# Attention ahead of two expert layers: GpSimd's low halves in pairs, projections two groups together, result turns ahead of both outputs

## The reference

```python
def _attn_ref(q, k, v, omega):              # q, k, v: 4 x 8 x 576 x 64, omega: 128 x 64
    scale = 1.0 / np.sqrt(np.sqrt(D))
    q_s, k_s = (q * scale, k * scale)
    def phi(x):
        proj = np.einsum('bhsd,md->bhsm', x, omega)
        h = proj - np.sum(x * x, axis=-1, keepdims=True) / 2.0
        h = h - np.max(h, axis=-1, keepdims=True)
        return np.exp(h) / np.sqrt(m)
    q_p, k_p = (phi(q_s), phi(k_s))
    kv = np.einsum('bhsm,bhsd->bhmd', k_p, v)
    z = np.sum(k_p, axis=2)
    num = np.einsum('bhsm,bhmd->bhsd', q_p, kv)
    den = np.einsum('bhsm,bhm->bhs', q_p, z)[..., None] + 1e-06
    return num / den
# x = attention, 2304 x 512
# x = (h * sigmoid(1.702 h)) @ w_out, h = x @ w_in      (512 -> 2048 -> 512)
# x = top-1 of 8 experts, relu(x @ w1[e]) @ w2[e]        (512 -> 1024 -> 512)
```

## Time and profile before

| | us |
|---|---|
| median of 3 runs | 808.28 (808.04 to 808.32) |
| the profiled execution | 808.37 |
| its span | 806.3 |
| unit 0 and the start, to the first `sums` | 12.56 |
| rest of step 0 | 9.94 |
| step 1 | 8.19 |
| loop, steps 2 to 13 | 109.04 |
| steps 14 and 15 to the first matmul of the next part | 13.21 |
| the two following parts | 653.4 |

### The profile page before, as it was taken

One profiled execution on the slowest core, in us unless ns is written; L12 is line 12 of the kernel. 1 busy time (PEld: TensorE's weight loads), 2 busy tenths in 40 slices (PEclk: granted clock), 3 DMA queues, 4 the chain that ended last, 5 costly groups with the idle time before them and its releaser, 6 DMA issues.

```text
span 806.3 us, 15801 instructions
## 1 busy us (share of the span) xinstructions
PE 776.8 (96%) x5514; PEld 711.9 (88%) x5515; DVE 361.1 (45%) x908; ACT 307.6 (38%) x714; POOL 322.1 (40%) x280
## 2 busy tenths in 40 slices
PE   7999989999999999999999999999999999999995
PEld 6777777889899989988989998997999999999994
DVE  5777777511224424433443445766763322331321
ACT  3777776633232232232233223253214324425320
POOL 5777776135322222212222223234026716627521
PEclk9999999999999999999999999999999999999998
DMA  8776674011050020010002001051062541621011
GB/s 298 288 253 229 240 267 158 1 53 53 1 183 0 1 78 0 0 49 29 0 0 78 0 0 40 21 199 33 28 221 77 162 144 47 216 72 39 29 59 31
DMA packets 25444, 74.17 MB, mean 92 GB/s; under 512 B 3120, under 2 KB 3632, under 8 KB 25280
## 3 DMA queue, kind: packets, MB, share of 16 engines
q1 hardware_dynamic: 22144, 63.68, 22.6%
q0 software_dynamic: 3264, 10.03, 4.1%
HBM read 61.11 MB, written 12.58 MB: 91 GB/s over the span
## 4 chain that ended last, share of the span: by engine, by line
PE 83%; ACT 4%; POOL 4%; issue 4%; DVE 3%; DMA 1%; SPq 0%; POOLq 0%; ACTq 0%; DVEq 0%
PE pj L701 25%; PE nm L883 16%; PE pj L1301 8%; PE kv L883 8%; PE kv L1317 6%; PE nm L1317 6%; PE nm L1301 5%; POOL sqt L205 2%; POOL sqt L201 2%; ACT feat L417 1%; PE pj L255 1%; PE pj L1330 1%; PE kv L273 1%; PE tr L1288 1%; ACT qfT L397 1%
## 5 line engine op out<-in xcount | busy, mean ns | idle before, releaser
L857 POOL TENSOR_TENSOR gl<-g,gh 128x384 fp32r<-128x384 f32 x96 | 99.2, 1036 | 306.6 <-ACT gh L719 306.6
L714 DVE TENSOR_TENSOR g<-pj,sg 128x384 f32<-128x384 f32 x96 | 53.5, 557 | 220.1 <-ACT sg L709 219.8
L709 ACT ACTIVATE sg<-pj 128x384 f32<-128x384 f32 x96 | 47.2, 492 | 254.1 <-PE pj L701 254.1
L701 PE MATMUL pj<-xh,win_h 128*128 128x384 f32 x384 | 129.5, 337 | 1.2 <-DVE xl L736 1.2
L701 PE MATMUL pj<-xh,win_l 128*128 128x384 f32 x384 | 129.4, 337 | 0.0
L701 PE MATMUL pj<-xl,win_h 128*128 128x384 f32 x384 | 128.9, 336 | 0.0
L701 PEld LDWEIGHTS pj<-xh,win_h 128*128 128x128 f32 x384 | 72.1, 188 | 5.2 <-DVE xl L736 1.5
L701 PEld LDWEIGHTS pj<-xl,win_h 128*128 128x128 f32 x384 | 72.1, 188 | 3.6
L701 PEld LDWEIGHTS pj<-xh,win_l 128*128 128x128 f32 x384 | 72.0, 188 | 0.0
L1301 PE MATMUL pj<-xTh,W 128*128 128x288 f32 x320 | 71.6, 303 | 0.0
L825 DVE SCALAR_TENSOR_TENSOR raw<-tr,xT 128x512 f32<-128x512 f32 x90 | 58.6, 688 | 8.2 <-DVE g L714 7.6
(11 more groups left out here) (255 smaller groups left out, 1695.4 us busy)
## 6 DMA issues: line engine op xcount, KB each, us to landing
wraw<-in_moe_w SPq DMA_DIRECT2D x7, 2048.0 KB, 10.9
ve<-in_v_z SPq DMA_DIRECT2D x16, 585.0 KB, 3.8
qk<-in_qk_n SPq DMA_DIRECT2D x16, 576.0 KB, 5.0
qkT<-in_qk_t SPq DMA_DIRECT2D x15, 576.0 KB, 5.4
y_rows<-ys SPq DMA_DIRECT2D x18, 256.0 KB, 2.3
stage<-in_moe_w_in SPq DMA_DIRECT2D x8, 512.0 KB, 6.2
y_early<-ys SPq DMA_DIRECT2D x12, 256.0 KB, 2.7
stage<-in_moe_w_out SPq DMA_DIRECT2D x4, 512.0 KB, 6.6
```

The lines of the kernel that those rows point to most:

```text
L701: mm = eng.matmul(ph[f % 3][:, 0:BT], w[f // F1A][:, c, f % F1A, :], x[:, c, :], start=(c == 0 and w is win_h and x is xh), stop=(c == DC ...
L709: eng.activation(sg[f % 2][:, :], ph[f % 3][:, 0:BT], ACT.Sigmoid, scale=1.702).then_inc(a_sg, 1)
L714: eng.tensor_tensor(g32[f % 2][:, :], ph[f % 3][:, 0:BT], sg[f % 2][:, :], ALU.mult).then_inc(v_g, 1)
L857: eng.tensor_tensor(gl[f % 3][:, :], g32[f % 2][:, :], gh[f % 3][:, :].bitcast(F32), ALU.subtract).then_inc(g_gl, 1)
```

## The change

- SyncE: unit 0's normal layout also comes in three pieces of 192 KB, each behind the piece of the turned layout of the same group. Both layouts of unit 1 come before the values of units 0 and 1. A load of `qk` waits no longer for VectorE's sums of the unit two before (`v_sq`) but for GpSimd's first squaring of it (`g_s0`, `g_sq`).
- GpSimd: in an even step only `squares`; in an odd one `squares` and then both `low` of the two steps.
- TensorE: `project(1)` directly behind `project(0)` and ahead of `sums`; all three `turn_x` ahead of both outputs; 5, 3 and 2 idle matmuls in place of 4, 4 and 4.
- ScalarE: in even steps from 2 on `copy_x(1)` and `copy_qf(2)` go ahead of `exps_b(1)`, and `copy_x(2)` ahead of `exps_a(1)`.
- VectorE: `norms` goes from the end of step i (for unit i + 2) into `front`, behind the first `top` of the unit that uses it.

```diff
@@ sync @@
+            if isinstance(i, int) and i == 2:
+                eng.wait_ge(g_s0, PG)
+            elif not isinstance(i, int) or i > 2:
+                eng.wait_ge(g_sq, 4 * (i - 3) + 1 if isinstance(i, int) else 4 * i - 11)
-            need(eng, v_sq, i - 1)
...
+        def first(g):
             n = GT * P
             eng.dma_start(qkT[0][:, GT * g:GT * g + GT, :].rearrange("p t c -> p (t c)"),
                           qk_t[0, :, g * n:(g + 1) * n]).then_inc(ld_0[g], 16)
+            n = 2 * GT * HD
+            eng.dma_start(qk[0][:, 2 * GT * g:2 * GT * (g + 1), :].rearrange("p j d -> p (j d)"),
+                          qk_n[0, :, g * n:(g + 1) * n]).then_inc(ld_1[g], 16)
...
+        eng.dma_start(om_r[:, :], om_2).then_inc(ld_om, 16)
+        for g in range(PG):
+            first(g)
+        load(1, 0, 1, None)
         for i in (0, 1):
-            load(i, 0, i, None)
+            values(i, i)
@@ gpsimd step @@
-            if chunk is not None:
-                low(i, n, a, chunk)
+            if chunk is not None and a == 1:
+                low(2 * n, n, 0, chunk)
+                low(i, n, 1, chunk)
@@ tensor @@
-        idle(4)
+        idle(5)
...
-        idle(4)
+        idle(3)
         project(0, 0, 0, 2)
-        idle(4)
+        idle(2)
@@ tensor step @@
             project(*x, 0)
+            project(*x, 1)
             sums(i, n, a)
-            project(*x, 1)
...
-            output(i, n, a, 0)
             if before:
                 turn_x(n - 1, 2, i)
+            output(i, n, a, 0)
             output(i, n, a, 1)
@@ scalar step @@
             copy_qf(i, n, a, 1, before)
+            if before:
+                copy_x(n - 1, 1)
+                copy_qf(i, n, a, 2, before)
             exps_b(*x, 1)
             if before:
-                copy_x(n - 1, 1)
-            copy_qf(i, n, a, 2, before)
+                copy_x(n - 1, 2)
+            else:
+                copy_qf(i, n, a, 2, before)
             exps_a(*x, 1)
-            if before:
-                copy_x(n - 1, 2)
@@ vector front @@
             if w:
                 denom(*w, 0)
+            if not isinstance(x[0], int) or x[0]:
+                norms(*x)
             top_h(*x, 0)
@@ vector step @@
-                else:
-                    norms(*y)
```

More of the change, by code:

```diff
@@ L113, in attention @@
     ld_om = sem("ld_om")
-    ld_0 = [sem(f"ld_0{g}") for g in range(PG)]
+    ld_0, ld_1 = ([sem(f"ld_{b}{g}") for g in range(PG)] for b in range(2))
     g_id = sem("g_id")
@@ L142, in load @@
         def load(i, n, a, chunk):
-            if isinstance(i, int) and i == 0:
-                eng.dma_start(om_r[:, :], om_2).then_inc(ld_om, 16)
-                first_t(0)
-            need(eng, v_sq, i - 1)
+            if isinstance(i, int) and i == 2:
+                eng.wait_ge(g_s0, PG)
+            elif not isinstance(i, int) or i > 2:
+                eng.wait_ge(g_sq, 4 * (i - 3) + 1 if isinstance(i, int) else 4 * i - 11)
             eng.dma_start(qk[a][:, :, :].rearrange("p j d -> p (j d)"),
@@ L152, in load, with values @@
             need(eng, p_pj, PG * (i - 1))
-            if isinstance(i, int) and i == 0:
-                for g in range(1, PG):
-                    first_t(g)
-            else:
-                eng.dma_start(qkT[a][:, :, :].rearrange("p t c -> p (t c)"),
-                              qk_t[bass.ds(i, 1), :, :].rearrange("i p r -> (i p) r")).then_inc(ld_t[a], 16)
+            eng.dma_start(qkT[a][:, :, :].rearrange("p t c -> p (t c)"),
+                          qk_t[bass.ds(i, 1), :, :].rearrange("i p r -> (i p) r")).then_inc(ld_t[a], 16)
             if chunk is not None:
                 weights(i - 2, a, chunk)
+            if not (isinstance(i, int) and i == 1):
+                values(i, a)
+        def values(i, a):
             need(eng, p_kv, i - 1)
@@ L163, in load @@
                           v_z[bass.ds(i, 1), :, :].rearrange("i p r -> (i p) r")).then_inc(ld_v[a], 16)
-        def first_t(g):
+        def first(g):
             n = GT * P
@@ L197, in squares @@
         def squares(i, n, a):
-            eng.wait_ge(ld_qk[a], 16 * (n + 1))
+            need(eng, ld_qk[a], 16 * (n + a))
             need(eng, g_sq, 4 * i - 4)
@@ L221, in step @@
                 squares(i + 2, n + 1, a)
-            if chunk is not None:
-                low(i, n, a, chunk)
-        eng.wait_ge(ld_qk[0], 16)
+            if chunk is not None and a == 1:
+                low(2 * n, n, 0, chunk)
+                low(i, n, 1, chunk)
         for g in range(PG):
+            eng.wait_ge(ld_1[g], 16)
             t = slice(2 * GT * g, 2 * GT * (g + 1))
@@ L583, in step @@
         def step(i, n, a, last):
-            w, x, y = (i - 1, n + a - 1, 1 - a), (i + 1, n + a, 1 - a), (i + 2, n + 1, a)
+            w, x = (i - 1, n + a - 1, 1 - a), (i + 1, n + a, 1 - a)
             if not last:
@@ L604, in vector @@
         front((0, 0, 0), None)
-        norms(1, 0, 1)
         half_steps(eng, step)
```

## The result

| | before | changed |
|---|---|---|
| median, beside each other (7 and 7 runs) | 808.28 | 803.79 (803.37 to 807.05) |
| a second time (7 and 4 runs) | 807.95 | 804.07 (803.68 to 804.17) |
| ratio, with its 95% interval | | 0.9961 (0.995 to 0.9973); second time 0.995 (0.9934 to 0.9967) |

Three of its seven first runs took 805.8 to 807.1 us, at a mean granted clock of 0.991 or 0.992, and four took 803.4 to 803.8 at 0.995 or 0.996. The profiled execution of that set was the slowest of them (807.05, span 805.2); one profile more, of the second set, has a span of 802.3. I use the second for the times of the stages, and the first for its clock and for one even step (its steps agree with those of the second to 0.01 us).

What follows compares the result with a forecast made beforehand. TensorE was taken to bound the attention loop, busy 99.8 of 109.0 us. The terms - 2.2 - 1.7 + 2.1 + 0.1 + 0.3 = - 1.4 us, on a span of 806.3, gave a median of 806.9 us, range 805.4 to 809.0.

Steps and rivals of the forecast that it cites:

- even steps: about nothing: Attention loop, even steps: 1.7 us gained from the division's wait, set against 2.1 us lost by the third result turn.
- The wait for the division: Even steps: TensorE's waits for VectorE's last division go, through GpSimd's paired lows and the moved norms; gain 1.7 us.
- The third turn: Even steps: the third result turn waits 0.38 us for a copy, 1.30 from turn to turn; loss 2.1 us.
- `project(1)` in odd steps: Odd steps: it needs the even step's last exponentials earlier, with slack 0.05 us; loss 0.1 us for all.
- Rival (c): Odd steps: ScalarE ends the last exponentials late and the two projections stop TensorE; up to 810.0 us, chance 0.11.
- The end: Last steps: the split of the first block stands behind a later third copy; loss 0.3 us.
- The start: Ahead of step 1: step 1 starts at 20.3 us and not 22.50; gain 2.2 us, bounds 0.5 to 2.5.
- (1): Start, unit 0: the first 192 KB land sooner, so its last exponentials end at 13.0 us, not 13.33.
- (3): Start, unit 1: squares start at 8.8 us, norms end at 13.9, exponentials end at 15.5, 1.1 us ahead of `project(2)`.
- The rule on small loads: Start: the skill page's advice to batch loads; six small ones would move unit 1 back some 4 us, chance 0.02.
- Rival (a): Start: TensorE's idle time makes the clock fall again, losing 0.7 to 1.7 us; about 808.1 us, chance 0.22.
- Rival (b): Loop and start: faster copies, third turns lose 1.2 us, odd steps keep VectorE's gain, start gives 2.5; 805.7 us, chance 0.13.

Runs made afterwards that it cites:

- e11: The changed kernel with one full-row matmul, a transpose of the identity, added right ahead of `project(1)`: 810.51 us in one run, step 1 8.29 us.
- e4: The changed kernel with TensorE's and ScalarE's order of a step as before: 805.26 us, ratio 0.9972 to the kernel before.
- e8: The changed kernel with the result turns and ScalarE's copies in the order of before: 803.37 us, ratio 0.9945 to the kernel before.
- e3: The changed kernel with `project(1)` behind `sums` again: 806.83 us, ratio 0.9983 to the kernel before.
- e2: The kernel before with the third result turn ahead of both outputs and ScalarE's copies in the changed order: 809.53 us, ratio 1.0023.
- e1: The kernel before with `project(1)` directly behind `project(0)`, ahead of `sums`, in all steps: 807.13 us, ratio 0.9994.

## Why the prediction was wrong

**The step that failed: "even steps: about nothing" and step 1 left as it was, since TensorE's own time was taken as fixed.** The six even steps of the loop were forecast at + 0.4 us together and measured at - 2.3, step 1 at nothing and measured at - 0.35, the six odd ones at + 0.1 and + 0.5. I took TensorE's own time as fixed and moved only waits. A projection that stands by itself costs 0.87, two together 1.54: 0.20 less. `sums` between two projections costs 2.21, followed by a transpose 2.12: 0.09 less. The transposes between two projections cost 0.48, behind `sums` 0.42: 0.06 less. In step 1, which has no result turns, these 0.35 are the whole difference, 8.19 to 7.84, in each of the eight profiles with the projections together and nothing between and in none without. It stood in the profile: step 1 had a projection in three places, and the earlier trace rows show its 0.94 each time. I read the 0.07 between 0.94 and 0.87 as an error of the modelled end, and never asked what a neighbour of the same kind would give. e11 shows it as a cost of the change-over; that it is the half rows and not another trait of these matmuls is argued, not shown. In the sum the pair of projections stood at nothing. By e4 and e8 it is worth 3.0 us, and the whole miss, - 1.4 forecast against - 4.0 between the spans, is 2.6.

**The wait for the division: nearly the right size, half of the reason wrong.** - 1.7 us in the loop forecast, - 1.2 measured with the norms alone, - 1.3 in e4. The first turn came at 5.41 from the step's start in e4, and not at my 5.30. I gave GpSimd's pairs a share in it. With the norms alone and GpSimd's order as before, the squares of a unit end at 66.75 and the norms use them at 67.50, and VectorE's 12 waits for squares (15.4 us between 30 and 135 us) are gone: the place of the norms is enough.

**The third turn: direction right, size too large.** + 0.38 per even step forecast, + 0.14 measured (4.05 to 4.19 from e4 to e3), as the third turn follows after 1.22 and not 1.30, and as the 36 matmuls of the outputs take 1.20 in one piece where they took 0.73 and 0.61 in two. The loop's loss is 0.95 with the projections apart (e3 against e4), 1.6 on the kernel before (e2) and 1.7 with the projections together (e8 against the changed kernel), not 2.1.

**`project(1)` in odd steps: mechanism right, size wrong.** I put a slack of 0.05 (by my own figures, 5.29 less 5.2, it is 0.09) and 0.1 us for all. It is short by 0.37 per odd step (77.03 - 75.89 = 1.14 where 0.77, half of 1.54, would do), because TensorE, with the saving above, comes earlier than I had it and ScalarE does not. Rival (c) ran, and the kernel was faster all the same: the pair saves 0.35 per step and this eats it in odd ones.

**The end:** + 0.3 forecast, - 0.1 measured. The turns cost 0.34 there (12.76 in e8, 13.10 changed), where I had reckoned 0.37; the pair, which was not in my sum, gives 0.46 (e1 against before) or 0.44 (e8 against e4).

**The start: - 2.2 forecast, - 1.4 in the second profile, + 0.3 in the first.** Steps (1) and (3) failed here, both on the loads. In the second profile:

```profile
10.51 2.11 POOL L208 TENSOR_TENSOR sqt<-qk 128x1152 f32<-128x1152 f32 x1 [0.59 <-DMA qk<-in_qk_n]
...
11.94 0.94 PE L264 MATMUL pj<-om,qkT 64*128 64x128 f32 x12 [1.00 <-DMA qkT<-in_qk_t]
...
12.38 0.88 ACT L427 ACTIVATE feat<-pj,nb 128x128 f32<-128x128 f32 x3 [1.13 <-DVE nb L538]
...
13.41 0.94 PE L264 MATMUL pj<-om,qkT 64*128 64x128 f32 x12 [0.54 <-ACT feat L427]
...
15.59 0.30 DVE L500 TENSOR_REDUCE ssq<-sq 128x18 f32<-128x144 f32 x1 [1.70 <-POOL sq L216]
...
16.33 0.88 ACT L427 ACTIVATE feat<-pj,nb 128x128 f32<-128x128 f32 x3 [2.65 <-DVE nb L538]
...
17.36 0.94 PE L264 MATMUL pj<-om,qkT 64*128 64x128 f32 x12 [0.47 <-ACT feat L427]
```

(1) had unit 0's last exponentials end at 13.0, 0.3 sooner. They end at 12.38 + 0.88 = 13.26: the wait of 0.29 is gone, but the maxima ahead of it begin at 5.80 where it was 5.47. So `project(1)` starts at 13.41. (3) Unit 1's normal layout lands at 10.5, not at 8.8, though fewer bytes are ahead of it; over all profiles the squares of unit 1 begin at 9.97 to 10.85 with the new loads and at 10.29 to 11.49 with the old ones. Its turned layout keeps `project(0)` waiting until 11.94. The exponentials begin at 16.33, and `project(2)` waits 0.47 for them; my fallback, "had the load gained nothing", said 0.3, and in its reason, the norms behind the maxima, it was right: `project(2)` comes 0.7 us sooner than before (17.36 for 18.06), as with the norms alone. The other 0.7 of the 1.4 is the low stretch of 19 to 22 us that this profile doesn't have (3.76 us from `project(2)` to step 1, 4.44 before). I had priced that stretch at 1.7. Loads ran slower while the small pieces were in flight, 4 to 6 us:

```profile
4.00:6.00 2.00, 1.78 (x15) 1.42 (x14) 0.20 (x1) 0.00 (x0) 0.82 (x1) 1.00 0.86 239
```

239 GB/s where it was 346; 205 to 288 in the ten profiles with the new loads, 338 to 360 in the four with the old ones. The rule on small loads in the Trainium skill (DMA: Bandwidth & Descriptors, section Bandwidth), which I gave little, points the right way here: the start lost most of what the order of the loads had won. The size that I drew from it, an estimate of some 4 us, is not seen, and my own terms gave less: three pieces at 1.6 us in place of 576 KB in 1.5 us are 3.3. That it is the size of the pieces, and not their order or number, is argued; no run changes one without the others.

Rival (a) is real too, and I gave it too little with 0.22. A stretch at 0.50 between 11 and 20 us stands in eight of the ten profiles with the new start (loads and idle matmuls); of the four with the old start only that of the kernel before has one ahead of step 1, from about 19 to 22 us. Window 15 to 16 us of the first profile:

```profile
15.00:16.00 1.00, 1.00 (x8) 0.78 (x6) 0.88 (x4) 0.25 (x1) 0.24 (x1) 0.50 1.00 411
```

Its projections are slow at first as well: up to 10.9 us, twelve matmuls take 1.58 to 1.66 us each time, where before they took 0.94 from 6.4 us on. In e4 twelve take 1.65 at a granted clock of 0.50 (from 12.06 us), so this is the pace of 1.2 GHz. Step 1 then starts at 22.80. Of the 2.9 us between the two profiles of the changed kernel 1.7 lie here (0.6 ahead of `project(1)`, 1.1 from there to `project(2)`, in the low stretch) and 1.1 behind attention, where the window from 560 to 570 us reads 0.86 in the first and 1.00 in the second.

**The signs, and luck.** Both things by which I said that the forecast would show itself wrong came: the low clock in the first profile and the wait of `project(1)` in odd steps. Both make the kernel slower, and it was faster than forecast all the same; no sign of mine could have shown the saving that I had left out. The loop left its bounds of 0.5 us (107.19 for 109.04), and the waits for result copies were 12 and 4.4 us, not 14 and 5.5. Rival (b), the one that named a faster kernel (805.7), has the right side for reasons of which little is seen: the third turn follows after 1.22 in place of 1.30, and odd steps did not get shorter.

## What to carry to other kernels

Price a group of matmuls by its neighbours: read the same group behind one of its own kind and behind another kind before taking TensorE's time as given. An order that makes one engine quicker must be followed by the engine that feeds it: here one line moved on ScalarE took another 2 us out of the loop. And undo each edit alone: the best of five edits (the norms) did 2.9 us on its own, by the medians; two did nothing that could be seen; one (the early turns) cost 1.8. The fifth, the two projections together, did nothing clear of noise on its own and 3.0 us behind the norms: what an edit saves on the engine that bounds shows only when the wait behind it is gone.

## What the runs showed of the hardware

A change between projections (64 of 128 rows) and full matmuls costs TensorE about 0.1 us, with nothing in the list of waits to show it: a projection takes 0.87 us to the next full-row matmul and 0.77 to the next projection, `sums` 2.21 ahead of a projection and 2.12 ahead of a transpose, and one transpose between two projections 0.25 where it takes 0.14 in a row. In several profiles TensorE ran at the pace of 1.2 GHz until some 10 us after the start, while the clock column of the windows read 1.00: only the matmuls' own times (1.65 against 0.94 for twelve) told it. That the column knows no clock ahead of the first recorded change is my reading and not shown. A stretch at 0.50 of about 3 us cost the start 0.7 us (before) and 1.1 us (first profile), less than half of its length. Behind attention a window at 0.86 in place of 1.00 went with 1.1 us more.
